# Rounded keys spread over both partition halves by transfers within SBUF, from one packed load, instead of a second load and a VectorE copy

## What is computed

```python
def _attn_ref(q, k, v):
    B, H, S, D = q.shape
    q_pool = q.reshape(B, H, S // 2, 2, D).mean(axis=3)
    scores = 1.0 / np.sqrt(D) * np.matmul(q_pool, k.transpose(0, 1, 3, 2))
    scores = scores - np.max(scores, axis=-1, keepdims=True)
    attn = np.exp(scores)
    attn = attn / (np.sum(attn, axis=-1, keepdims=True) + 1e-09)
    return np.matmul(attn, v).astype(np.float32)
...
    x = np.ascontiguousarray(attn_out.transpose(0, 2, 1, 3)).reshape(B * S, H * D)
    x = _moe_ref(x=x, **moe_kwargs)        # h = x @ w_in; (h * tanh(softplus(h))) @ w_out
    return _moe2_ref(x=x, **moe2_kwargs)   # h = x @ w_in; elu(h) @ w_out
```

## Time and profile before

| what | value |
|---|---|
| median of 3 runs | 748.13 us |
| lowest and highest | 745.28 and 748.25 us |
| span of the profiled execution, its own time from the first to the last instruction | 746.8 us |
| mean granted TensorE clock in it | 0.973 |
| PE, DVE, ACT, POOL busy | 92%, 74%, 50%, 61% of the span |
| transfers | 54.72 MB, 40.37 MB of them read from HBM |

### The profile page before, as it was taken

How to read it: one execution, slowest core, us unless ns; L and a number is a source line. 1 busy time by engine, 2 the same in 40 slices (tenths; PEclk the granted TensorE clock), 3 DMA queues, 4 the chain that set the end, 5 groups by cost and what they waited for, 6 DMA issues and landing times.

```text
span 746.8 us, 13443 instructions
## 1 busy us (share of the span) xinstructions
PE 688.3 (92%) x4064; PEld 657.3 (88%) x4064; DVE 553.3 (74%) x791; ACT 371.8 (50%) x693; POOL 457.8 (61%) x390
## 2 busy tenths in 40 slices
PE   3999898979898989869999999999999999999998
PEld 2889797979797988868889999888899999999998
DVE  7788989898989898699999999999963323223222
ACT  2678686868786877733444333543353322121211
POOL 3486868686777787548777666777764442222221
PEclk9699999999999999989999999999999999999999
DMA  7454545455455542021110000121222201001001
GB/s 211 118 152 123 145 118 142 122 133 133 132 133 133 133 133 54 15 57 57 48 54 28 0 0 0 43 57 56 57 60 82 57 15 43 0 0 43 1 0 43
DMA packets 30373, 54.72 MB, mean 73 GB/s; under 512 B 4480, under 2 KB 11904, under 8 KB 30336
## 3 DMA queue, kind: packets, MB, share of 16 engines
q1 hardware_dynamic: 30336, 54.25, 26.9%
HBM read 40.37 MB, written 2.36 MB: 57 GB/s over the span
## 4 chain that ended last, share of the span: by engine, by line
PE 57%; DVE 24%; issue 12%; POOL 3%; ACT 1%; DVEq 1%; DMA 1%; SPq 0%; POOLq 0%; ACTq 0%
PE pm L370 6%; PE py L494 6%; PE py L496 6%; PE py L495 6%; PE pH L481 5%; PE pH L480 5%; PE pH L479 5%; DVE fi L839 5%; PE po L410 4%; PE ps L394 4%; PE po L411 3%; PE po L412 3%; PE ps L395 3%; DVE part_max L701 3%; DVE fe L822 2%
## 5 line engine op out<-in xcount | busy, mean ns | idle before, releaser
L1008 POOL TENSOR_TENSOR gl<-fg,gh 128x384 fp32r<-128x384 f32 x96 | 107.4, 1118 | 129.4 <-ACT gh L627 129.4
L948 POOL TENSOR_TENSOR pl<-p,ph 128x576 fp32r<-128x576 f32 x72 | 109.5, 1523 | 58.1 <-ACT p L567 54.5
L494 PE MATMUL py<-gh,wout_h 128*128 128x384 f32 x384 | 130.7, 340 | 10.3 <-POOL gl L1008 10.1
L701 DVE TENSOR_REDUCE part_max<-pm 128x1 f32<-128x384 f32 x231 | 125.0, 554 | 18.9 <-PE pm L370 12.2
L479 PE MATMUL pH<-xh,win_h 128*128 (+1 forms) x384 | 129.4, 337 | 6.1 <-DVE fg L816 6.1
L481 PE MATMUL pH<-xh,win_l 128*128 (+1 forms) x384 | 129.1, 336 | 0.0
L480 PE MATMUL pH<-xl,win_h 128*128 (+1 forms) x384 | 129.0, 336 | 0.0
L496 PE MATMUL py<-gh,wout_l 128*128 128x384 f32 x384 | 128.6, 335 | 0.0
L495 PE MATMUL py<-gl,wout_h 128*128 128x384 f32 x384 | 128.5, 335 | 0.0
L565 ACT ACTIVATE ph<-ps 128x576 fp32r<-128x576 f32 x144 | 93.9, 652 | 64.7 <-PE ps L395 61.6
L650 ACT ACTIVATE fe<-pH 128x384 f32<-128x384 f32 x95 | 46.1, 485 | 135.3 <-PE pH L481 135.1
(11 more groups left out here) (69 smaller groups left out, 1460.1 us busy)
## 6 DMA issues: line engine op xcount, KB each, us to landing
k_raw<-kT SPq DMA_DIRECT2D x32, 288.0 KB, 4.2
w_raw<-w_in SPq DMA_DIRECT2D x32, 256.0 KB, 2.9
w_raw<-w_out SPq DMA_DIRECT2D x32, 256.0 KB, 2.6
q_raw<-qT SPq DMA_DIRECT2D x16, 288.0 KB, 3.3
k_pack<-kP SPq DMA_DIRECT2D x16, 288.0 KB, 2.7
v_raw<-v SPq DMA_DIRECT2D x16, 288.0 KB, 2.7
kl<-k_pack SPq DMA_DIRECT2D x32, 144.0 KB, 4.4
q<-q_hi SPq DMA_DIRECT2D x62, 72.0 KB, 2.3
```

The lines of the kernel that those rows point to most:

```text
L494: pe.matmul(out, hi, gh[:, f % 4, :], start=(f == 0), stop=False)
L701: dve.tensor_reduce(part_max[:, par, t, c:c + 1], chunk_bank(j, par, first), AX.X, ALU.max).then_inc(m_read, 1)
L948: pool.tensor_tensor(pl[:, ph_slot(slot, kt), :], p32[:, kt % 3, :], ph[:, ph_slot(slot, kt), :].bitcast(F32), ALU.subtract).then_inc(pl_p ...
```

## The change

The load of `kT` and the tile `k_raw` go. DVE's `copy_kh` goes, for all heads. `k_hi`, which was made before only to form the remainder, is spread to both halves of `kh` by four transfers within SBUF of 64 partitions by 576 elements, placed in `spread_head` behind those of `q2`. Head 0 is spread by four DVE copies. `round_k` moves on ACT from behind the row of maxima in step 5 to step 2 (even heads) and 3 (odd heads), and waits for the spread of the head before; `split_k` moves on POOL from step 6 to 4 and 5.

```diff
-GPSIMD_AT = {"sum_q": (0, 0), "split_q": (3, 2), "split_k": (6, 6), "split_v": (1, 1), "split_w": (4, 4),
+GPSIMD_AT = {"sum_q": (0, 0), "split_q": (3, 2), "split_k": (4, 5), "split_v": (1, 1), "split_w": (4, 4),
              "multiply_sums": (1, None), "split_x": (None, 2)}
-SCALAR_AT = {"split_q": (4, 2), "split_v": (0, 1), "split_w": (3, 3)}
-VECTOR_AT = {"copy_kh": (7, 6), "invert": (4, None), "finalize": (6, None)}
+SCALAR_AT = {"round_k": (2, 3), "split_q": (4, 2), "split_v": (0, 1), "split_w": (3, 3)}
+VECTOR_AT = {"invert": (4, None), "finalize": (6, None)}
...
@@ SP: spread_head
                 for part, cols in ((top, slice(0, HQ)), (low, slice(HQ, SQ))):
                     move(q2[par][top, cols], q_hi[part, :]).then_inc(q2_spread, 16)
-                if not last:
-                    sp.wait_ge(kh_done, m + 1)
-                    load_k(m + 1)
+                if not (isinstance(m, int) and m == 0):
+                    sp.wait_ge(k_rounded, m + 1)
+                    for rows in (top, low):
+                        for part, cols in ((top, slice(0, HK)), (low, slice(HK, SK))):
+                            move(kh[par][rows, cols], k_hi[part, :]).then_inc(kh_spread, 16)
                 sp.wait_ge(kl_done, m + 1)
...
@@ PE: max_chunk
-                    wait(pe, kh_done, n + 1)
+                    wait(pe, kh_spread, 64 * (n + 1))
                     wait(pe, q1_spread, 64 * (n + 1))
@@ ACT: round_k
                 wait(act, kl_done, n)
+                wait(act, kh_spread, 64 * n)
                 act.activation(k_hi[:, :], k_pack[:, :], ACT.Copy).then_inc(k_rounded, 1)
...
@@ DVE
-            def copy_kh(n, par):
-
-                dve.wait_ge(k_in, 32 * (n + 1))
-                wait(dve, s_filled, slot_count(n - 2, KT - 1))
-                dve.tensor_copy(kh[par][:, :], k_raw[:, :]).then_inc(kh_done, 1)
...
-            copy_kh(0, 0)
+            dve.wait_ge(k_rounded, 1)
+            for rows in (slice(0, D), slice(D, 2 * D)):
+                for part, cols in ((slice(0, D), slice(0, HK)), (slice(D, 2 * D), slice(HK, SK))):
+                    dve.tensor_copy(kh[0][rows, cols], k_hi[part, :].bitcast(F32)).then_inc(kh_spread, 16)
```

More of the change, by code:

```diff
@@ L55, in wait, with build @@
     eng.wait_ge(sem, value)
-def build(nc, qT, kT, kP, v, w_in, w_out, outT):
-    HEADS, D, SK = kT.shape
-    HK = SK // 2
+def build(nc, qT, kP, v, w_in, w_out, outT):
+    HEADS, HK = kP.shape[0], kP.shape[2]
+    D, SK = kP.shape[1] // 2, 2 * HK
     SQ = 2 * qT.shape[3]
@@ L99, in build @@
             ident = sa("ident", [P, P])
-            k_raw = sa("k_raw", [P, SK])
             k_pack = sa("k_pack", [P, HK])
@@ L147, in build @@
         out_stage = [fn[:, d] for d in range(4)]
-        k_in, q_in, v_in = sem("k_in"), sem("q_in"), sem("v_in")
+        q_in, v_in = sem("q_in"), sem("v_in")
         w_rd = [sem(f"w_rd{i}") for i in range(2)]
@@ L157, in build @@
         sum_prod, sum_inv = sem("sum_prod"), sem("sum_inv")
-        kh_done, kl_done, vh_done, vl_done = sem("kh_done"), sem("kl_done"), sem("vh_done"), sem("vl_done")
+        kh_spread, kl_done, vh_done, vl_done = sem("kh_spread"), sem("kl_done"), sem("vh_done"), sem("vl_done")
         m_filled, m_read, max_ready = sem("m_filled"), sem("m_read"), sem("max_ready")
@@ L289, in load_q @@
                 sp.dma_start(q_raw[:, :, :], qT[m]).then_inc(q_in, 16)
-            def load_k(m):
-                for half in range(2):
-                    sp.dma_start(k_raw[half * D:half * D + D, :], kT[m]).then_inc(k_in, 16)
             def load_kp(m):
@@ L333, in _ @@
             load_q(0)
-            load_k(0)
             load_kp(0)
@@ L606, in pair_step @@
                             maxima_row(n + 1, 1 - par)
-                            if not in_last_pair(p):
-                                round_k(n + 2)
                         at = lambda task: SCALAR_AT[task][par] == kt
@@ L613, in pair_step @@
                             split_w(chunk(win_h, n), n, par)
+                        if at("round_k") and not in_last_pair(p):
+                            round_k(n + 2)
                         if at("split_q") and not in_last_pair(p):
@@ L762, in _ @@
             preset_v(0)
-            copy_kh(1, 1)
             preset_scores(1)
@@ L790, in pair_step @@
                         at = lambda task, step=kt: VECTOR_AT[task][par] == step
-                        if at("copy_kh") and not in_last_pair(p):
-                            copy_kh(n + 2, par)
                         if nxt is not None and kt < KT - 1 and nxt[1] in VKT[nxt[2]]:
@@ L1074 @@
         "qT": put(q.reshape(B * H, 2, SQ // 2, 2, D).transpose(0, 1, 4, 3, 2)).reshape(B * H, 2 * D, 2, SQ // 2),
-        "kT": put(k.reshape(B * H, S, D).transpose(0, 2, 1)),
         "kP": put(k.reshape(B * H, 2, S // 2, D).transpose(0, 1, 3, 2)).reshape(B * H, 2 * D, S // 2),
@@ L1083 @@
     outT = nc.dram_tensor("outT", (DM, B * SQ), F32, kind="ExternalOutput").ap()
-    build(nc, t["qT"], t["kT"], t["kP"], t["v"], [t["w_in0"], t["w_in1"]], [t["w_out0"], t["w_out1"]], outT)
+    build(nc, t["qT"], t["kP"], t["v"], [t["w_in0"], t["w_in1"]], [t["w_out0"], t["w_out1"]], outT)
     r = run_bass_kernel_spmd(nc, [arrays], core_ids=[0])
```

## The result

The changed kernel takes 764.8 us (median of 4 runs, 763.0 to 765.6) against 746.8 (median of 4, 745.3 to 748.3) beside it: 2.4% longer, ratio 1.0243, 95% interval 1.0216 to 1.027, so 18 us. The forecast was 757, with 743 to 771 as its range. (The span of the profile before and the median beside this run are the same number by chance. A run's time is some 1.9 us above its span: the profiled run of the changed kernel has 763.0 and 761.2.)

What follows compares the result with a forecast made beforehand. PE, busy in nearly all of the attention, stalls when kh arrives late from DVE's copy. Terms 2.5 + 1.1 + 3.7 + 2.25 = +9.6 us on the profiled 746.8 make 756.4, given as 757; range 743 to 771.

Steps and rivals of the forecast that it cites:

- Landing and chain: SP's transfers to kh: 1.8 us of issue, 2.35 landing, 0.2 to PE's start; chunks 4.35 us behind the q2 transfers.
- Head 0's end, +2.5: At head 0's end, where DVE's copy was in time, a new PE stall of 2.5 us for kh.
- The start, 0: PE's first matmul: earlier packed keys against four copies and ACT; taken as zero, bounds -1.5 and +1.5 us.
- Even heads, +3.7: Ends of heads 2 to 12: six stalls grow from 2.2 to some 2.8 us, 0.62 each, +3.7 us.
- Odd heads, +2.25: Ends of odd heads: first just hidden, three later ones late by under 1 us each, together +2.25 us.
- round_k and split_k at nothing: The moved steps on ACT and GpSimd fall into idle time there, so they cost nothing.
- The clock, +1.1: Behind head 0's new stall the clock halves for 3.3 us, costing 1.1 us; seven stretches at 0.50, one more.
- DVE's busy time, some 19 us less: Expected sign: without the copies, DVE's busy time in the attention falls by some 19 us.
- near no change: Rival: even boundaries cost only +0.3 each, odd ones hidden, head 0's stall does not halve the clock; 750 us, chance 0.20.
- faster: Rival: the spread is in before PE asks, so 12.9 us of waits and clock losses go; 728 us, chance 0.13.

Runs made afterwards that it cites:

- the best order: Changed kernel with kh ahead of q2 and of the next queries' load, and split_k back at step 6: 740.4 us, 0.9899 of before.

## Why the prediction was right, and where its sizes were off

The sign, the mechanism and the place were right: a wait for the spread took the place of the wait for the copy, and grew. The kernels with kh 1.24 us sooner and 1.24 us later (-16 and +23 us) show it; the rest is sizes. By the prediction's own steps:

- *Landing and chain.* 2.35 us of landing: measured 2.5. The issue of four: 2.4 reckoned, 2.52 as a rule, but 2.92, 3.24, 3.56 and 3.72 at four of the fifteen. 4.35 us from the end of the q2 transfers to the chunks: 4.4 to 4.6, and 4.9 to 5.8 where the issue was slow. The estimate of 2.34 us from the Trainium skill's rule (DMA: Bandwidth & Descriptors, Anatomy of one DMA) was near the row. Landings grow with the bytes in the profile: 2.2 us for 72 KB, 2.5 for 144 KB, 2.6 to 2.7 for 256 KB and 2.8 to 3.2 for 288 KB. By that rule, which is stated for GpSimd's path, an estimate of them is 2.17, 2.34, 2.60 and 2.68, so the trace agrees but for the top of the last.
- *Head 0's end, +2.5.* The stall came, 2.49 us. But head 0 itself was shorter: the place was 2.1 us later than before, and 1.5 of this is the start. So the term was +0.6. Two things go with this, neither tested alone: a copy left DVE's list early in head 0, and the clock was at its lower level there for some 3 us less (its mean was 0.80 over 18 to 44 us, against 0.75 over 18 to 45 us before).
- *The start, 0.* +1.5, at the bound. Four CASTs took 4.28 us, 1.05 each, where the shortest took 0.454: GpSimd's split_k and split_v ran beside them from 5.80 to 9.61 us.
- *Even heads, +3.7.* The six waits were 14.8 us together against 12.9: +1.9. I had 2.8 us for each; they were 1.70 to 3.76, the longest where the two transfers to q2 took 2.26 us to issue and not 1.2.
- *Odd heads, +2.25.* This is the term that was mis-sized most. I had three of seven late, by under 1 us. Six waited, 6.6 us together (0.91, 0.89, 1.14, 2.34, 0.92, 0.40 at the ends of heads 3 to 13), so 4.4 more than reckoned. The ends of heads 3 and 5 had the slow issue: PE asked 4.8 and 4.9 us behind the q2 transfers, which a chain of 4.6 would have met. At the ends of heads 7 and 9 PE asked for kh sooner, 17.4 and 17.0 us behind the first chunks at the end before, against 19.4 and 18.4 in the kernel before. These stretches began with a fall of the clock before and with none now. SP's chain started only 0.8 and 0.3 us sooner, so what PE had gained was spent waiting. Where the clock fell in both traces, PE asked as before: 18.3 and 18.2 us against 18.4 and 18.2 (heads 11 and 13).
- *round_k and split_k at nothing.* For round_k that held. For split_k it held in this kernel only because kh covers it: PE's waits for part_max grew from 8.1 to 11.5 us and fell to 9.1 with the move undone, but the time did not; where kh is sooner the move costs 4 us.
- *The clock, +1.1.* Seven falls were forecast, one more than before. There were five stretches at half clock behind ends of heads, one of them of 7 us. Together they are some 20 us, as the six before, so this term came to nothing.
- *DVE's busy time, some 19 us less.* It fell by 2.2 us (553.3 to 551.1). The copies gave back 19.7 us, but the four CASTs took 4.2 and the subtractions pl grew by 11.6, from 1.06 to 1.23 us each; they stand at 1.14 with split_k alone undone. Undoing that gave no time here, but the change did not free DVE as I had said.

Waits for kh beyond head 0's (+8.5), start (+1.5), head 0 (+0.6) and part_max (+3.4) make 14.0 of the 14.4 us between the traces, where I had 9.6. The terms that were too small miss 9.3 us (odd heads 4.4, part_max 3.4, start 1.5) and those that were too large 4.8 (head 0, even heads, clock). So half of the misses cancelled, and that the total came as near as it did is in part luck.

The other 3.6 us of the measured 18 are the choice of executions: the profiled run of the changed kernel was the fastest of its four, 1.8 us under their median, and a span of 746.8 stands for a run of some 748.7, 1.9 over the median beside it. The prediction had taken that span for a run's time on the way from 756.4 to 757.

The rival "near no change" needed a chain 0.4 to 0.9 us shorter; the kernel with 1.24 us less takes as long as the one before. The rival "faster" had its ceiling at 728; the kernel without copies puts it at 735, and the best order at 740.4.

## What to carry to other kernels

Taking a copy off a busy engine gives nothing when the next stage waits for the moment at which its data arrive, and the new way there is no shorter: ask what the data's last hop stands behind, in the queue that issues it. The transfers within SBUF here went out one by one and cost 0.6 us of issue each, so the ones that the next stage reads first go first; here two lines in another order were worth 16 us. An edit that looks free while something else is last must be tried again once that is gone: split_k's place was worth 0 before and 4 us after.

## What the runs showed of the hardware

The granted clock did not follow the length of a stall as I had thought. In the kernel before each stall of 2.2 us at an even head's end was followed by 3.3 us at half clock. In the changed kernel windows behind two stalls of 2.35 and 2.60 us are at full clock; one behind 1.71 us is not, though one of 1.70 us (at 165.85) was followed by no fall either (columns as in the earlier trace rows):

```profile
84.00:90.00 6.00, 4.51 (x27) 4.05 (x28) 4.78 (x7) 3.57 (x7) 4.10 (x4) 1.00 0.50 140
...
204.70:210.00 5.30, 5.22 (x35) 4.95 (x36) 4.70 (x10) 5.29 (x10) 2.51 (x3) 1.00 0.50 132
...
243.50:248.00 4.50, 3.80 (x16) 3.81 (x17) 2.17 (x5) 2.74 (x6) 2.23 (x3) 0.62 0.68 189
```

What decides between them stays open. The falls also differ from one execution to the next: the mean granted clock of the kernel before was 0.973 to 0.991 over its runs. The other surprise is SP's issue: the same transfer of 64 by 576 took 0.6 us as a rule and up to 1.8. The long ones came in the first 145 us alone; their cause is not known:

```profile
L281 SPq DMA_DIRECT2D kh<-k_hi x60: 472/597/1805, 17.7 to 300.1; - x60
```
